# Fixed first row, clearing from SyncE, an earlier tail, filler matmuls and nested branches in an attention + two-MoE kernel

## What is computed

```python
# q, k, v: 4 x 8 heads x 576 rows x 64; tau 0.02
scores = q @ k.T / 8;  keep scores >= rowmax - tau
x = softmax(kept scores) @ v           # -> x: 2304 tokens x 512
# first MoE: 8 experts, 512 -> 1024 -> 512, top-1
logits = normalise(x) @ normalise(expert_emb).T / moe_tau
e = argmax(logits);  gate = softmax(logits)[e]
x = gate * (relu(x @ w1[e]) @ w2[e])
# second layer: 512 -> 2048 -> 512
h = x @ w_in;  out = (max(h, 0) + alpha * min(h, 0)) @ w_out
```

## Time and profile before

| | us |
|---|---|
| median of 3 runs | 1079.95 (1078.45 to 1081.27) |
| the profiled execution | 1076.72, its span 1075.0 |
| attention and routing up to PE's last small matmul | about 372 |
| slot 0's first weight matmul | 384.92 |
| last slot's work done, second layer begins | about 655 |
| mean granted clock of TensorE | 0.986 of full |

### The profile page before, as it was taken

How to read it: one execution, slowest core, us unless ns; L and a number is a source line. 1 busy time by engine, 2 the same in 40 slices (tenths; PEclk the granted TensorE clock), 3 DMA queues, 4 the chain that set the end, 5 groups by cost and what they waited for, 6 DMA issues and landing times.

```text
span 1075.0 us, 19435 instructions
## 1 busy us (share of the span) xinstructions
PE 1014.5 (94%) x6493; PEld 890.3 (83%) x6494; DVE 532.3 (50%) x1206; ACT 382.6 (36%) x812; POOL 346.1 (32%) x453
## 2 busy tenths in 40 slices
PE   6999999999999569999999997999999999999997
PEld 5888888888888558888888886999999899999996
DVE  5687887788887611222111214654444444434442
ACT  4566666666665322322232322221121111211211
POOL 2133334312112399799957272001010010100101
PEclk9999999999999879999999999999999999999999
DMA  6466677657644266546555345100001000000000
GB/s 170 113 147 140 151 187 188 165 148 193 146 104 120 86 220 199 199 160 201 197 174 161 118 151 167 53 1 30 30 31 30 1 29 29 29 0 0 30 1 29
DMA packets 102858, 116.30 MB, mean 108 GB/s; under 512 B 70269, under 2 KB 70301, under 8 KB 102277
## 3 DMA queue, kind: packets, MB, share of 16 engines
q1 hardware_dynamic: 86884, 84.49, 29.1%
q0 software_dynamic: 4928, 17.23, 4.5%
q10 hardware_dynamic: 10976, 13.67, 4.0%
HBM read 68.53 MB, written 18.82 MB: 81 GB/s over the span
## 4 chain that ended last, share of the span: by engine, by line
PE 64%; DVE 2%; issue 1%; ACT 1%; DMA 1%; POOL 1%; ACTq 0%; POOLq 0%; DVEq 0%
PE bank L679 60%; PE bank L682 3%; POOL x_sorted L613 0%; DMA x_row<-x_sorted 0%; ACT exps L1038 0%; DVE probs L1272 0%; DMA x_sorted<-zero_row,zero_pos 0%; DVE neg_max L1261 0%; DVE ring L1563 0%; DVE xT_lo L1523 0%; DVE X L1304 0%; DVE y_row L1532 0%; POOLq L84 0%; ACT xT_hi L1117 0%; ACT ring L1196 0%
## 5 line engine op out<-in xcount | busy, mean ns | idle before, releaser
L679 PE MATMUL bank<-x_hi,ring 128*128 128x384 f32 x768 | 211.9, 339 | 3.1 <-DVE act L1621 3.1
L679 PE MATMUL bank<-ring,g_hi 128*128 128x512 f32 x576 | 179.1, 392 | 0.0
L1204 ACT ACTIVATE g_hi<-act 128x384 fp32r<-128x384 f32 x96 | 50.4, 525 | 304.0 <-DVE act L1621 301.5
L574 POOL TENSOR_TENSOR ring<-stage,ring 128x2048 fp32r<-128x2048 f32 x32 | 147.2, 4599 | 4.7
L679 PEld LDWEIGHTS bank<-x_hi,ring 128*128 128x128 f32 x768 | 141.2, 189 | 6.9 <-DVE act L1621 3.4
L1038 ACT ACTIVATE exps<-bank,neg_max 128x576 f32<-128x576 f32 x144 | 102.1, 741 | 111.3 <-DVE neg_max L1261 111.3
L1618 DVE TENSOR_SCALAR neg<-bank,alpha_col 128x384 f32<-128x384 f32 x96 | 59.1, 616 | 145.4 <-PE bank L679 145.4
L679 PE MATMUL bank<-x_lo,ring 128*128 128x384 f32 x384 | 129.5, 337 | 0.0
L679 PEld LDWEIGHTS bank<-ring,g_hi 128*128 128x128 f32 x576 | 106.8, 188 | 18.7 <-DVE g_lo L1569 0.3
L1272 DVE SCALAR_TENSOR_TENSOR probs<-bank,thresh,exps 128x576 f32<-128x576 f32 x144 | 112.5, 814 | 14.5 <-ACT exps L1038 9.6
L679 PE MATMUL bank<-k_st,q_st 128*128 128x288 f32 (+5 forms) x696 | 112.6, 311 | 4.8 <-DVE probs L1272 3.4
(11 more groups left out here) (183 smaller groups left out, 1422.4 us busy)
## 6 DMA issues: line engine op xcount, KB each, us to landing
stage<-in_moe_w SPq DMA_DIRECT2D x32, 1024.0 KB, 5.3
k_st<-k_both SPq DMA_DIRECT2D x60, 288.0 KB, 4.8
x_row<-x_sorted ACTq DMA_DIRECT2D x23, 296.0 KB, 3.2
y_sorted<-y_row ACTq DMA_DIRECT2D x21, 256.5 KB, 2.6
q_st<-q_hi SPq DMA_DIRECT2D x30, 160.0 KB, 3.0
q_st<-q_lo SPq DMA_DIRECT2D x30, 160.0 KB, 3.3
qraw<-in_q SPq DMA_DIRECT2D x16, 256.0 KB, 3.2
vraw<-in_v SPq DMA_DIRECT2D x16, 256.0 KB, 4.8
```

Of the source, the lines that this page charges most:

```text
L574: nc.gpsimd.tensor_tensor(lo, src, hi.bitcast(F32), ALU.subtract).then_inc(piece_lo, 2)
L679: return nc.tensor.matmul(dst, lhsT, rhs, start=start, stop=stop)
L1204: nc.scalar.activation(g_hi[f % 3][:, :], act2[f % 2][:, :], ACT.Copy).then_inc(g_hi_ready, 1)
```

## The change

Slot 0's rows are read from row 0 of `x_sorted` and not from where the table says, and without waiting for the table. The clearing DMAs go from POOL's queue to SP's, as direct DMAs at a row that SP loads from `zero_at` (eight whole numbers on one partition in place of the 128 x 8 of `zero_pos`). The last tail is normalised ahead of routing group 3, and its two stores go out on two queues. PE gets 26 matmuls of 512 columns on one piece of weights, into a bank that nothing reads again. The last slot's number and expert are loaded ahead of the slots. The loop and branches behind slot 17 become seven written-out copies of the body, each inside the branch of the one before, so that a false branch leaves all of them. Behind the last slot that these inputs fill, three copies are left out by it, 277 rows of PE's listing.

```diff
+WARM = 26
 def for_slots(eng, body):
-            with eng.Fori(MIN_SLOTS, SLOTS - 1) as i:
-                with eng.If(i < end - 1):
-                    body(i, True)
-            with eng.If(end > SLOTS):
-                body(SLOTS - 1, False)
+            def rest(i):
+                with eng.If(end > i + 1):
+                    body(i, i + 1 < SLOTS)
+                    if i + 1 < SLOTS:
+                        rest(i + 1)
+            rest(MIN_SLOTS)
 # SP
             sp.wait_ge(x_ready, UNITS * PAIRS)
-            store_tail(PAIRS - 1)
+            store_tail(sp, PAIRS - 1, (0,))
+            sp.wait_ge(route_const, 8)
+            sp.dma_start(x_sorted[EXPERTS * CAP:...], zero_row ...).then_inc(zeroed[2], 16)
+            sp.wait_ge(zero_ready, 1)
+            for e in range(EXPERTS):
+                row = sp.value_load(zero_at[0:1, e:e + 1], ...)
+                sp.dma_start(x_sorted[ds(row, P), :], zero_row[:, :]).then_inc(zeroed[min(e, 2)], 16)
 # POOL, behind the last scatter
-            pool.wait_ge(zero_ready, 1)
-            for e in range(EXPERTS):
-                pool.indirect_dma_start(x_sorted, ..., zero_row[:, :], None).then_inc(zeroed[min(e, 2)], 16)
-            pool.dma_start(x_sorted[EXPERTS * CAP:...], zero_row ...).then_inc(zeroed[2], 16)
 # PE
             rank(4)
+            pe.wait_ge(piece_lo, PIECES)
+            for _ in range(WARM):
+                mm(bank[:, M_BANK, :], ring[:, 0, 0:P], ring[:, 0, 0:D], True, True)
 def slot(i, more):
                 e, half_at = expert_of(i)
+                if static(i):
+                    turn_slot(0)
             pe.wait_ge(table_ready, 1)
-            turn_slot(0)
-            for_slots(pe, slot)
             last_slot = pe.value_load(slot_count[0:1, 1:2], ...)
             e_last, half_last = expert_of(last_slot)
+            for_slots(pe, slot)
 # ACT
-            act.wait_ge(table_ready, 1)
+            act.wait_ge(x_ready, UNITS * PAIRS)
+            store_tail(act, PAIRS - 1, (1,))
             act.wait_ge(scattered, 16 * TT)
             act.wait_ge(zeroed[0], 16)
-            row = act.value_load(slot_row[0:1, 0:1], ...)
-            act.dma_start(x_row[:, :], x_sorted[ds(row, P), :]).then_inc(xs_in, 16)
+            act.dma_start(x_row[:, :], x_sorted[0:P, :]).then_inc(xs_in, 16)
             ...
             act.wait_ge(zeroed[1], 16)
+            act.wait_ge(table_ready, 1)
             load_slot(1)
 # DVE
             normalise(PAIRS - 1, UNITS - 2)
+            normalise(PAIRS - 1, UNITS - 1)
             for k in range(7):
                 route_step(3, k)
-            normalise(PAIRS - 1, UNITS - 1)
-            V.tensor_scalar(zero_pos[:, :], total, iota_p[:, 0:1], None, ALU.add).then_inc(zero_ready, 1)
+            V.tensor_copy(zero_at[:, :], total[0:1, :]).then_inc(zero_ready, 1)
```

More of the change, by code:

```diff
@@ L122, in build @@
         slot_count = at("slot_count", [1, 2], I32)
-        zero_pos = at("zero_pos", [P, EXPERTS], U32)
+        zero_at = at("zero_at", [1, EXPERTS], I32)
         alpha_col = at("alpha_col", [P, F2C])
@@ L166, in build @@
         iota_int = at("iota_int", [P, TABLE], I32)
-        iota_pint = at("iota_pint", [P, 1], I32)
-        iota_p = at("iota_p", [P, 1])
         iota_e = at("iota_e", [P, EXPERTS])
@@ L443, in spread_k, with store_tail @@
                                   k_both[head, :, :].bitcast(F32)).then_inc(spread_in[par], 16)
+        def store_tail(eng, n, heads):
+            t, at_p = TAIL_TILES[n // 8], TAIL * (n // 4 % 2)
+            for h in heads:
+                at_x = t * XC + n % 4 * TURNED + h * (TURNED // 2)
+                eng.dma_start(X[at_p:at_p + TAIL, at_x:at_x + TURNED // 2],
+                              x_tail_sb[h * TAIL:(h + 1) * TAIL, :]).then_inc(tail_stored, 16)
         block = ctx.enter_context(nc.Block())
@@ L462, in load_v @@
                              view[:, MAIN * P:SEQ, :].rearrange("h r d -> r h d")).then_inc(v_in[par], 16)
[L464 to L469, removed]
             load_q(sp, 1, 1)
@@ L498, in body @@
                     sp.wait_ge(x_ready, UNITS * n)
-                    store_tail(n - 1)
+                    store_tail(sp, n - 1, (0, 1))
             for n in range(PAIRS):
@@ L509, in _ @@
             sp.wait_ge(x_ready, UNITS * PAIRS)
-            store_tail(PAIRS - 1)
+            store_tail(sp, PAIRS - 1, (0,))
+            sp.wait_ge(route_const, 8)
+            sp.dma_start(x_sorted[EXPERTS * CAP:EXPERTS * CAP + 2 * P, :].rearrange("(i p) n -> p i n", p=P),
+                         zero_row[:, :].rearrange("p (o n) -> p o n", o=1).to_broadcast([P, 2, XC])).then_inc(zeroed[2], 16)
+            sp.wait_ge(zero_ready, 1)
+            for e in range(EXPERTS):
+                row = sp.value_load(zero_at[0:1, e:e + 1], min_val=0, max_val=EXPERTS * CAP)
+                sp.dma_start(x_sorted[ds(row, P), :], zero_row[:, :]).then_inc(zeroed[min(e, 2)], 16)
             load_expert(1, 4)
@@ L554, in _ @@
             nc.gpsimd.iota(iota_int[:, :], pattern=[[1, TABLE]], base=0, channel_multiplier=0)
-            nc.gpsimd.iota(iota_pint[:, :], pattern=[[1, 1]], base=0, channel_multiplier=1)
             x_meta = X[:, :].rearrange("p (t n) -> p t n", n=XC)[:, :, XL + EXPERTS].bitcast(I32)
@@ L624, in _ @@
                     scatter(t)
-            pool.wait_ge(route_const, 8)
-            pool.wait_ge(zero_ready, 1)
-            for e in range(EXPERTS):
[L628 to L631, removed]
             split_pieces(1, 1, 0, PIECES)
@@ L1167, in store_y @@
                 act.dma_start(y_sorted[ds(at_y, P), D + 1:YC], x_sorted[ds(row, P), XL:XL + META]).then_inc(y_stored, 16)
-            act.wait_ge(table_ready, 1)
+            act.wait_ge(x_ready, UNITS * PAIRS)
+            store_tail(act, PAIRS - 1, (1,))
             act.wait_ge(scattered, 16 * TT)
             act.wait_ge(zeroed[0], 16)
-            row = act.value_load(slot_row[0:1, 0:1], min_val=0, max_val=EXPERTS * CAP)
-            act.dma_start(x_row[:, :], x_sorted[ds(row, P), :]).then_inc(xs_in, 16)
+            act.dma_start(x_row[:, :], x_sorted[0:P, :]).then_inc(xs_in, 16)
             split_slot(0)
@@ L1457, in constants @@
                 V.memset(iota_k[:, 0:1], -1.0)
-                V.tensor_copy(iota_p[:, :], iota_pint[:, :])
                 V.tensor_scalar(base_e[:, :], iota_int[:, 0:EXPERTS], float(CAP), None, ALU.mult)
```

## The result

The changed kernel takes 1091.49 us (median of 4 runs, 1090.41 to 1094.08) beside 1079.2 for the kernel before on the same chip (4 runs, 1076.49 to 1081.27): a ratio of 1.0119, 95% interval 1.0088 to 1.015. Forecast was 1077.0. The span of the profiled execution is 1088.8 against 1075.0.

A forecast was written before the change was run, and what follows sets the result against it. PE, busy 94% of the span, left only waits or low-clock stretches to gain from. Rows 1.25, transposes 0.5 and clock 1.2 sum to 2.95; 1079.95 - 2.95 = 1077.0, range 1075.1 to 1080.1.

The forecast's parts named there:

- The failed step: POOL's queue without the clearing DMAs: ten freed microseconds worth nothing, as PE never waits for POOL there; 256-row clearing charged 0.
- The register loads at 0: Four PE register loads between table and slot 0's transposes, ending 377.85 to 380.65, covered by the rows' load: cost 0.
- The clearing from SP: SP's clearing DMAs run beside the fifth scatter: 0.3 added to its landing, with bounds 0 and 0.76.
- The rival in which the clearing delays the rows by 2.75: Slot 0's rows land behind all eight clearings, at 384.6: 1.05 slower, 1081.0; chance 0.12.
- The tail: Tail normalised ahead of group 3: group 3 and POOL's scatters 0.82 later, the table 0.64 earlier.
- The row term: Slot 0's rows, loaded without waiting for the table, land at 380.6: 1.25 earlier (0.5 to 1.6).
- The transposes: Slot 0's transposes on PE, after filler, take 0.60 and not 1.10: gain 0.5.
- The filler's end: 26 filler matmuls on PE from 371.7 end at 379.2 to 379.6, 1.0 to 1.4 before the rows.
- The clock term: Slot 0's weight matmuls at full clock for part of the time: gain 1.2, of 2.16 if kept throughout.
- falls again fully: Rival: PE's clock falls again fully ahead of slot 0; gain 1.75, time 1078.2; chance 0.15.
- The branch at 0: PE's forward branch behind the last slot costs 0; at most one 2.6 fetch, hidden in the wait for y.
- Its sign of being wrong: PE's wait behind the last slots well over 2.4 would show the forecast wrong.

The follow-up runs named there:

- the kernel without filler: The kernel with both repairs, less the 26 filler matmuls ahead of slot 0's transposes: 1080.41 us, ratio 1.0012 to the kernel before.
- both repairs: Changed kernel with POOL's split of expert 1's weights waiting for the slot table, and the old loop restored behind slot 17: 1078.16 us, ratio 1.0002.
- moving the split alone: Changed kernel, but POOL splits expert 1's weights only once the slot table is written: 1078.94 us, ratio 1.0004 to the kernel before.
- the dose kernel: Changed kernel with the old loop behind slot 17; POOL runs only its split's first instruction beside the table, then waits for it: 1079.47 us, ratio 1.0002.

## Why the prediction was wrong

**The failed step** is "POOL's ten freed microseconds are worth nothing: PE never waits for it in this stage. That clearing is charged at 0." PE indeed does not wait for POOL there; DVE does, through no semaphore. (In the two kernels with the split moved and filler on one side the profile puts slot 0's last wait, 1.75 and 1.78, down to POOL. The pieces that PE needs there were there before the filler began, and the kernel without filler has the same 1.75 behind DVE's `xT_lo`.) The step asked who waits for the split and not what runs beside it once it moves. Slot 0 came 9.14 later than before and 10.58 later than with both repairs (30.14 and 19.56 behind the mark), and moving the split alone brings the ratio from 1.0119 to 1.0004. The split of before did not show the price: the DVE instructions beside it read a PSUM bank, but for copies of one SBUF element a partition (`ssq_slot`, 0.14), and none was stretched (ns, minimum, median, maximum):

```profile
L1523 DVE TENSOR_TENSOR xT_lo<-bank,xT_hi x22: 690/692/692, 383.8 to 645.3; 128x512 fp32r<-128x512 f32 x22
```

But the trace of before did hold the collision the other way round, behind the last slots. POOL's `tau_ok` has one element a partition, as have some of its `row_eps`; beside DVE's instruction on `ring` and `stage`, two inputs in SBUF, it took four times as long:

```profile
659.37 0.80 POOL L656 TENSOR_TENSOR tau_ok<-zero 128x1 f32<-128x1 f32 x1 [11.62 <-DMA y_sorted<-x_sorted]
L602 POOL TENSOR_TENSOR row_eps<-row_sum,guard x80: 189/195/198, 17.4 to 359.2; 128x2 f32<-128x2 f32 x64, 128x1 f32<-128x1 f32 x16
658.89 2.36 DVE L1563 TENSOR_TENSOR ring<-stage,ring 128x1024 fp32r<-128x1024 f32 x2 [2.70 <-ACT ring L1196]
L1563 DVE TENSOR_TENSOR ring<-stage,ring x8: 1220/1226/1227, 658.9 to 683.3; 128x1024 fp32r<-128x1024 f32 x8
```

The first of DVE's two ends at 658.89 + 1.22 = 660.11 and POOL's at 660.17; in every trace of this study POOL's ends 0.05 behind DVE's, whenever it started. With that sign, and POOL's instructions 1.9 and 4.6 long beside a chain of tiny ones, the step could have been given a bound: four of them fit beside the table.

**The register loads at 0** fell with it. Their cover was the load of the rows; the step named them as the next wait if that came sooner. It was the table that came later, and 2.95 lay bare, inside the 1.2 to 4.0 given. In the dose kernel, with the table at 377.91, they are the last wait too: PE starts at 381.49 behind 3.04 of "issue", 4.61 behind ACT's issue of the rows at 376.88, where the kernel with both repairs needs 3.57.

**The clearing from SP** at its 0.3: in the kernel with both repairs ACT issues 3.45 behind the fifth scatter's start, in the others with this clearing 3.27 to 4.13, against 377.25 - 374.01 = 3.24 in the forecast. The term was too small by 0.03 to 0.9, in most kernels by 0.2 to 0.5. The rival in which the clearing delays the rows by 2.75 is not seen.

**The tail** went as computed: the fifth scatter 10.12 behind the mark, forecast 374.01 - 363.92 = 10.09. In three of the other kernels with the tail ahead it is the same, in four it is 10.5 to 10.6. That sum said itself that the scatters come 0.82 later; undoing it, with filler unchanged, took the ratio from 0.998 to 0.9961.

**The row term** of 1.25: with both repairs the transposes start 17.15 behind the mark, 18.07 before: 0.92. **The transposes** gave 0.43 of 0.5. **The filler's end** was forecast 7.5 to 7.9 behind its start; by the forecast's own numbers (3.1 to 4.1 at half clock, the rest at 0.2335 each) it is 7.6 to 8.1. It was 7.85 in the changed kernel and 7.84 to 8.69 over the six with 26 matmuls.

**The clock term** of 1.2 was worth nothing on average. Two kernels have the forecast's case, filler on one side and the table on time, and do not differ up to slot 17: the one with the split moved and the one with both repairs. In both the clock fell at about 383.4, just ahead of slot 0, the rival "falls again fully", to which I gave 0.15. It came back at about 386.9 in one and 390.2 in the other, so the 24 matmuls took 7.29 and 8.57, against 7.76 before: 0.5 gained and 0.8 lost. Over all six kernels with 26 filler matmuls they took 7.29 to 8.57, 7.75 in the mean. With both repairs slot 1's transposes come 27.96 behind the mark, 0.63 sooner than before in place of 2.95; with the split moved, 1.47 sooner. Behind the last slots the clock then fell in both pauses, where the profiled execution of before kept it in the first. With both repairs 1.6 went there (14.74 from the last product's start to the end of the second layer's first wait, 13.17 before). That is where the forecast's gain went in that execution: of 2.95, 0.6 came, and the clock's falls further on took it back. One execution shows one pattern of falls; what the 12 runs share is the ratio of 1.0002. The prediction's mean of 0.95 over 364.6 to 369.0 should have been 0.96, as in the row. Its range ends at 1080.1, where its own sum gives 1079.4 + 0.5 = 1079.9.

**The branch at 0**: the stall of 4.25 to 4.60 lies above the upper bound of one fetch, 2.6, and under the 6.2 from which it was to decide by itself. Its sign of being wrong, a wait behind the last slots well over 2.4, did not show in the changed kernel (2.39), where no loads stand behind the branch; it did in the kernel with the nested branches alone (3.73). The prediction weighed the Trainium skill, "Runtime: NRT & Kernel Launch", section "Instruction fetch mechanics", against the row of the backward jump, and took the row. The forward jump did stall, as the page says. A row of another jump was no measure of this one.

**Chances and range**: a slower kernel had 0.06, from mishaps that were each known. An instruction stream that moves ten microseconds beside another engine's critical chain was in none of the cases.

## What to carry to other kernels

When work leaves a queue, list what moves up behind it and lay that beside every engine that works in the new place, not only beside those that wait for it by a semaphore. A chain of tiny DVE instructions with two inputs in SBUF, or of tensor_scalar there, is a bad neighbour for POOL's long ones. A wait on POOL for the end of the chain gave back some 12.5 here. A tiny instruction that takes several times its usual length, and ends with a long one of another engine that it has no semaphore with, is the sign to look for in the trace of before. Filler matmuls held the clock here when they stood on both sides of the small work ahead of the heavy matmuls (four kernels of four); on one side they did not (none of six).

## What the runs showed that I had not expected

- A DVE instruction of 32 elements took 6.92 us beside POOL's memsets; its recorded start lay 0.2 behind POOL's there, and beside the split up to 0.5 ahead of it (373.70 and 374.19).
- A taken forward branch on PE, out of four written-out bodies, took 4.25, 4.33 and 4.60 us in three kernels; the same branches not taken took 0.07 to 0.08, and a forward jump over one body in the loop 0.21.
- With the same instructions in the same places, whether the clock falls in a pause of 2.39 behind the slots, or just after it, differs: it was kept in the profiles of five kernels, the one before (2.38) among them, and lost in those of four, the one with both repairs among them. 11 small matmuls in the pause kept it in both kernels that had them.
